# A three-stage kernel (decayed linear attention, routed experts, dense MLP): w, k and r laid out head-dimension first

## The reference

```python
# B, H, S, D = 4, 8, 768, 48
for t in range(S):                              # attention
    cur = einsum('bhd,bhe->bhde', u * k[t], v[t])
    y[t] = einsum('bhd,bhde->bhe', r[t], state + cur)
    state = w[t][..., None] * state + einsum('bhd,bhe->bhde', k[t], v[t])
x = y as (B*S, H*D) = (3072, 384)
# 8 experts: noisy top-2 routing, out += weight * relu(x @ w1[e]) @ w2[e]
# then h = x @ w_in ; out = (h - tanh(h)) @ w_out
```

## Time and profile before

| | us |
|---|---|
| median of 3 runs | 1186.56 (1183.66 to 1186.65) |
| profiled execution, time | 1191.79 |
| profiled execution, span | 1190.3 |
| PE busy | 1104.0 (93%) |
| DVE busy | 738.1 (62%) |
| ACT busy | 567.3 (48%) |
| POOL busy | 136.8 (11%) |

### The profile page before, as it was taken

The page is one execution under the profiler, slowest core; times in us unless marked ns, Lnnn a source line. Parts: engine busy times, 40 slices in busy tenths (PEclk is TensorE's granted clock), DMA queues, the critical chain, the costliest instruction groups (busy, mean ns, idle before and its releaser), DMA issues.

```text
span 1190.3 us, 24896 instructions
## 1 busy us (share of the span) xinstructions
PE 1104.0 (93%) x8968; PEld 1053.2 (88%) x8968; DVE 738.1 (62%) x1036; ACT 567.3 (48%) x808; POOL 136.8 (11%) x188
## 2 busy tenths in 40 slices
PE   5888867789799999999999999999999999999998
PEld 4677756689799999999999999899999999999998
DVE  8999988638957777766677777643434333343433
ACT  5445433346347666666666666532332323333232
POOL 1000223212820000000000000221010101101010
PEclk9999889889999999999999999999999999999999
DMA  9664555556778888888888888511010101101010
GB/s 154 122 123 88 121 117 157 175 189 190 258 245 288 280 278 269 281 277 276 276 273 289 264 276 282 184 47 36 25 60 0 59 0 59 59 0 59 0 59 20
DMA packets 192751, 185.04 MB, mean 155 GB/s; under 512 B 98192, under 2 KB 160912, under 8 KB 192688
## 3 DMA queue, kind: packets, MB, share of 16 engines
q1 hardware_dynamic: 176208, 152.74, 44.8%
q0 software_dynamic: 6528, 20.06, 5.1%
q10 hardware_dynamic: 9952, 11.41, 2.8%
HBM read 156.85 MB, written 27.33 MB: 155 GB/s over the span
## 4 chain that ended last, share of the span: by engine, by line
PE 77%; DVE 13%; issue 5%; ACT 3%; SPq 1%; POOL 1%; DMA 1%; another core or an unknown queue 0%; DVEq 0%; ACTq 0%; POOLq 0%
PE ps L789 6%; PE ps L858 6%; PE ps L876 6%; PE ps L878 6%; PE ps L877 6%; PE ps L859 6%; PE ps L860 6%; PE ps L790 5%; PE ps L791 5%; PE ps L747 5%; PE ps L749 4%; PE ps L748 4%; PE ps L767 2%; PE ps L766 2%; PE ps L765 2%
## 5 line engine op out<-in xcount | busy, mean ns | idle before, releaser
L1590 DVE TENSOR_TENSOR w_lo<-w_raw,w_hi 128x1536 fp32r<-128x1536 f32 x140 | 244.3, 1755 | 93.3 <-ACT w_hi L909 88.1
L909 ACT ACTIVATE w_hi<-w_raw 128x1536 fp32r<-128x1536 f32 x140 | 206.5, 1488 | 24.8 <-ACT y_out L1101 12.3
L1590 DVE TENSOR_TENSOR gg<-ps,th 128x768 f32<-128x768 f32 x64 | 61.3, 957 | 168.3 <-ACT th L1148 168.3
L789 PE MATMUL ps<-w_hi,h_hi 128*128 128x384 f32 x440 | 151.0, 343 | 9.0 <-DVE h_lo L1674 8.3
L747 PE MATMUL ps<-xT_hi,w_hi 128*128 128x256 f32 x480 | 139.6, 291 | 10.9 <-issue 5.7
L791 PE MATMUL ps<-w_hi,h_lo 128*128 128x384 f32 x440 | 147.9, 336 | 0.0
L790 PE MATMUL ps<-w_lo,h_hi 128*128 128x384 f32 x440 | 147.9, 336 | 0.0
L1878 POOL DMA_INDIRECT yy<-yg,slot_g x54 | 54.2, 1004 | 751.3 <-DVE w_lo L1590 425.5
L749 PE MATMUL ps<-xT_hi,w_lo 128*128 128x256 f32 x480 | 137.2, 286 | 0.0
L748 PE MATMUL ps<-xT_lo,w_hi 128*128 128x256 f32 x480 | 137.1, 286 | 0.0
L876 PE MATMUL ps<-wout_hi,g_hi 128*128 128x384 f32 x384 | 130.4, 340 | 0.0
(11 more groups left out here) (266 smaller groups left out, 2088.1 us busy)
## 6 DMA issues: line engine op xcount, KB each, us to landing
w_raw<-in_moe_w SPq DMA_DIRECT2D x140, 768.0 KB
xt_in<-xg SPq DMA_DIRECT2D x20, 384.0 KB
yg<-y_out ACTq DMA_DIRECT2D x20, 384.0 KB
k_pad<-in_k SPq DMA_DIRECT2D x32, 144.0 KB, 3.9
v_nat<-in_v SPq DMA_DIRECT2D x32, 144.0 KB
out<-o_out SPq DMA_DIRECT2D x8, 576.0 KB
w_nat<-in_w SPq DMA_DIRECT2D x15, 288.0 KB, 3.3
r_pad<-in_r SPq DMA_DIRECT2D x30, 144.0 KB
```

The costliest lines, as they stand in the source:

```text
L789: pe.matmul(o, h_hi[:, f, cols], w2_hi[:, f, :], start=(f == 0), stop=False, skip_group_check=True)
L909: nc.scalar.activation(dst, src, ACT.Copy).then_inc(s, 1)
L1590: vec.tensor_tensor(dst, a, b, ALU.subtract).then_inc(s, 1)
```

## The change

The host passes w, k and r a second time with the head dimension before time, and v with the two heads of a pair together. k and r are loaded straight into klin and rlin, w straight into wz, which is now double. `turn`, `straight`, `spread_in`, `squares` and `see` go away. Padding rows of klin and rlin are cleared once by POOL, wz is set to 1 once by DVE.

The scores of a chunk are made in 64-step blocks: the upper-right part that the mask would clear is not computed. DVE masks only the two diagonal 64x64 blocks of each chunk (`mask`, 384 elements a partition into Ad), and ACT copies the off-diagonal one (`apart`, into Ao). `intra` multiplies the diagonal blocks and a new `below` the off-diagonal ones. The betas go to the KV bank. The bonus rows are added on PE, as two matmuls with the identity (`add_bonus`), and ACT instead of DVE copies the finished rows (`tokens`). The range check of w is two Relu instructions on ACT with an accumulated sum (`check_range`). `finish` (the wait for a batch's last rows and the branch to the general path) moves from place 3 of pairs 3, 7 and 11 to place 0 of the next pair. The cast of the first w1 also waits for the last kr.

```diff
+wz = two(place, "wz", [P, Q * W1 + 1])
...
+def load_cols(e, dst, src, landed, n, h):
+    s = n % 2
+    e.dma_start(dst[s][h * HB:h * HB + D, :], src[n // HP, 2 * (n % HP) + h]).then_inc(landed[s], 16)
+
+def load_w(e, n, h):
+    s = n % 2
+    e.dma_start(wz[s][h * HB:h * HB + D, 0:Q * W1].rearrange("d (q s) -> d q s", s=W1)[:, :, 1:W1],
+                w_cols[n // HP, 2 * (n % HP) + h].rearrange("d (q s) -> d q s", s=C)).then_inc(w_in_s[s], 16)
...
 def next_w(n):
 
     if n < NP:
-        sp.wait_ge(spread, n - 1)
-        sp.wait_ge(w_squared, n - 1)
-        load_w(n)
+        sp.wait_ge(scanned, 2 * (n - 2) + 2)
+        sp.wait_ge(w_checked, 2 * (n - 2) + 2)
+        for h in range(2):
+            load_w(sp, n, h)
...
+        c0 = (t * QT + j) * C
+        pe.matmul(ps[0:HB, A0 + h, j * C:(j + 1) * C], kG[s][rows, c0:c0 + HB], rPW[s][rows, c0:c0 + C], start=True, stop=True)
+        mm = pe.matmul(ps[HB:C, A0 + h, j * C:j * C + HB], kG[s][rows, c0 + HB:c0 + C], rPW[s][rows, c0 + HB:c0 + C],
                        start=True, stop=True)
-if t == 0:
-    mm.then_inc(A_full, 1)
+mm.then_inc(A_full, 1)
...
+pe.matmul(ps[rows, KV, BETA + 2 * q:BETA + 2 * q + D], kr[:, q * C + half * HB:q * C + (half + 1) * HB],
+          usel[:, p % HP, :], start=True, stop=True, skip_group_check=True)
...
+                o = (h * QT + q % QT) * HB
+                mm = pe.matmul(ps[rows, Y0 + h, q * D:(q + 1) * D], Ad[q // QT][rows, o:o + HB], v_nat[s][rows, q, h, :],
+                          start=(q == 0), stop=(q == 0), skip_group_check=True)
+    mm.then_inc(diagonal, 1)
+
+def below(p):
+
+    s = p % 2
+    pe.wait_ge(diagonal, p + 1)
+    for q in range(Q):
+        for h in range(2):
+            o = (h * QT + q % QT) * HB
+            mm = pe.matmul(ps[HB:C, Y0 + h, q * D:(q + 1) * D], Ao[q // QT][:, o:o + HB], v_nat[s][0:HB, q, h, :],
+                           start=False, stop=True, skip_group_check=True)
     mm.then_inc(intra_done, 1)
+
+def add_bonus(p):
+
+    pe.wait_ge(bv_done, p + 1)
+    for h in range(2):
+        pe.matmul(ps[:, Y0 + h, 0:Q * D], ident[:], bv[:, :, h, :], start=False, stop=True, skip_group_check=True)
...
 for p in range(NP):
     scores(1, p)
     if p % HP == 2:
         any_bad(p // HP)
     betas(p)
-    back(p)
     step(p, 0)
-    if p + 2 < NP:
-        turn(1, p + 2)
     outer(p)
     step(p, 1)
     intra(p)
     if p + 1 < NP:
         scores(0, p + 1)
+        back(p + 1)
+    below(p)
+    add_bonus(p)
     inter(p)
     step(p, 2)
-    if p + 2 < NP:
-        turn(2, p + 2)
-    if p + 3 < NP:
-        turn(0, p + 3)
     step(p, 3)
...
+def apart(t, p):
+
+    act.wait_ge(A_masked, 2 * p + t + 1)
+    follow(act, intra_done, p)
+    cp(Ao[t][:].rearrange("s (h j t) -> s h j t", h=2, t=HB),
+       ps[0:HB, A0:A0 + 2, 0:QT * C].rearrange("s h (j t) -> s h j t", t=C)[:, :, :, HB:C], A_apart)
+
+def tokens(p):
+
+    b, hp = p // HP, p % HP
+    act.wait_ge(Y_full, p + 1)
+    cp(x_all[b][:, :, hp * PW:(hp + 1) * PW].rearrange("t q (h d) -> t h q d", h=2),
+       ps[0:C, Y0:Y0 + 2, 0:Q * D].rearrange("t h (q d) -> t h q d", d=D), x_done)
...
+act.wait_ge(w_in_s[n % 2], 32 * (n // 2 + 1))
+values = wz[n % 2][:, 0:Q * W1].rearrange("d (q s) -> d q s", s=W1)[:, :, 1:W1]
+for side, sign in ((0, -1.0), (1, 1.0)):
+    follow(act, w_checked, 2 * n + side)
+    nc.scalar.activation(w_out_of[:].rearrange("d (q s) -> d q s", s=C), values, ACT.Relu, bias=limits[:, side:side + 1],
+                         scale=sign, accum_out=over[:, n, side:side + 1]).then_inc(w_checked, 1)
...
 for p in range(NP):
-    keep_back(p)
+    apart(0, p)
+    apart(1, p)
     step(p, 0)
-    straight(1, p + 2)
-    squares(p + 3)
+    chunk_products(p + 2)
     step(p, 1)
-    chunk_products(p + 2)
+    check_range(p + 3)
     step(p, 2)
-    straight(2, p + 2)
-    straight(0, p + 3)
-    spread_in(p + 4)
+    if p + 1 < NP:
+        keep_back(p + 1)
+    tokens(p)
     step(p, 3)
...
+vec.tensor_tensor(Ad[t][:].rearrange("s (h j t) -> s h j t", h=2, t=HB),
+                  ps[0:C, A0:A0 + 2, 0:QT * C].rearrange("s h (j t) -> s h j t", t=C)[:, :, :, 0:HB],
+                  before_h[:].unsqueeze(1).unsqueeze(1).to_broadcast([C, 2, QT, HB]), ALU.mult).then_inc(A_masked, 1)
...
 for p in range(NP):
     if p == 2:
         v_.wait_ge(tidied, TIDIED)
         v_.wait_ge(consts, 16 * (3 + H))
-    mask(0, p)
+    if p > 0:
+        mask(0, p)
     decayed_k(p + 1)
     step(p, 0)
     suffix_scan(p + 2)
     mask(1, p)
+    decayed_r(p + 1)
+    bonus(p)
     if p % HP == 2:
         range_all(v_, p // HP)
-    bonus(p)
     step(p, 1)
-    decayed_r(p + 1)
     states(p)
     step(p, 2)
     prefix_scan(p + 2)
     products(p + 1)
-    see(p + 3)
-    tokens(p)
     step(p, 3)
...
+po.memset(klin[0][:], 0.0).then_inc(zeroed, 1)
+po.memset(rlin[0][:], 0.0).then_inc(zeroed, 1)
...
+v_pairs = inputs["v"].reshape(B, HP, 2, Q, C, D).transpose(0, 1, 4, 3, 2, 5)
+for name, a in [(f"{n}_cols", inputs[n].transpose(0, 1, 3, 2)) for n in "rkw"] + [("v_pairs", v_pairs)]:
+    a = np.ascontiguousarray(a)
```

More of the change, by code:

```diff
@@ L196, in build @@
         badv = place("badv", [P, 8])
+        over = place("over", [P, NP, 2])
         bad_i = place("bad_i", [1, B, 2], I32)
@@ L684, in step @@
                     part()
-            pe.wait_ge(gaps, 1)
-            for which in range(3):
-                turn(which, 0)
-            turn(0, 1)
+            pe.wait_ge(setup, 1)
             scores(0, 0)
-            turn(1, 1)
-            turn(2, 1)
-            turn(0, 2)
+            back(0)
             for p in range(NP):
@@ L905, in _ @@
-            nc.scalar.activation(tick[:, 3:4], minus_mid[:], ACT.Copy)
-            act.wait_ge(gaps, 8)
+                load_cols(act, rlin, r_cols, r_in_s, 0, h)
+            act.wait_ge(wz_set, 6)
+            load_w(act, 1, 1)
+            act.wait_ge(zeroed, 4)
+            for h in range(2):
+                load_cols(act, rlin, r_cols, r_in_s, 1, h)
+            act.wait_ge(restarts, 5)
+            nc.scalar.activation(tick[:, 3:4], limits[:, 0:1], ACT.Relu)
             def cp(dst, src, s):
@@ L909, in cp @@
                 nc.scalar.activation(dst, src, ACT.Copy).then_inc(s, 1)
-            def straight(which, n):
-                if n >= NP:
-                    return
-                t = T_USE["wkr"[which], n]
-                if which == 0:
-                    follow(act, scanned, 2 * n)
-                else:
-                    follow(act, kr_r, n - 1)
-                    follow(act, (kG_r, rPW_r)[which - 1], n - 1)
-                for half in range(2):
-                    act.wait_ge(T_full[half], t + 1)
-                    src = ps[:, TB[half], 0:3 * P]
-                    if which == 0:
-                        dst = wz[:, 0:Q * W1].rearrange("d (q s) -> d q s", s=W1)[:, :, 1 + half:W1:2]
-                        src = src.rearrange("d (q p) -> d q p", q=Q)
-                    else:
-                        dst = (klin, rlin)[which - 1][n % 2][:, half * QT * C:(half + 1) * QT * C]
-                    nc.scalar.activation(dst, src, ACT.Copy).then_inc(T_copied[half], 1)
@@ L1002, in smooth, with first_high @@
                 ins.then_inc(sp_act, 1)
+            def first_high():
+                act.wait_ge(kr_r, NP)
+                for hf in range(2):
+                    w1_high(whole(0), hf)
             def kept(c, *places):
@@ L1538, in decayed_k @@
                     return
-                for half in range(2):
-                    v_.wait_ge(T_copied[half], T_USE["k", n] + 1)
+                v_.wait_ge(k_in_s[n % 2], 32 * (n // 2 + 1))
                 vec.tensor_tensor(c3(kG[n % 2][:]), c3(klin[n % 2][:]), w3(Gz[:])[:, :, 1:W1], ALU.mult).then_inc(kG_r, 1)
@@ L1545, in decayed_r @@
                     return
-                for half in range(2):
-                    v_.wait_ge(T_copied[half], T_USE["r", n] + 1)
+                v_.wait_ge(r_in_s[n % 2], 32 * (n // 2 + 1))
                 v_.wait_ge(scanned, 2 * n + 2)
@@ L1816, in _ @@
                                  pattern=[[1, C]], channel_multiplier=-1))
+            for h in range(2):
+                half = slice(h * HB, (h + 1) * HB)
+                seq(po.affine_select(out=before_h[half, :], in_=ones[half, 0:HB], compare_op=ALU.is_gt, fill=0.0, base=0,
+                                     pattern=[[1, HB]], channel_multiplier=-1))
+            po.memset(klin[1][:], 0.0).then_inc(zeroed, 1)
+            po.memset(rlin[1][:], 0.0).then_inc(zeroed, 1)
             seq(po.iota(part_no[:], pattern=[[0, 1]], base=1, channel_multiplier=1, allow_small_or_imprecise_dtypes=True))
```

252 lines of the change are left out of this document (90 added, 162 removed).

## The result

The changed kernel takes 1200.08 us (median of 4 runs, 1199.52 to 1203.78), the kernel before 1185.83 (median of 4, 1183.66 to 1186.65): ratio 1.0125, 95% interval 1.0106 to 1.0144. It is slower by 1.2%; forecast were 1158.5 us. Its profiled execution took 1203.78 us, its span 1202.3, 12.0 us more than before.

A forecast was written before the change was run, and what follows sets the result against it. DVE, 90% busy, was taken to bound the attention pairs. Savings of 13.8 (pairs 0 to 7), 11 (pairs 8 to 15) and 3.3 (start), 28.1 us off 1191.79, gave 1163.7, as median 1158.5 us; range 1149 to 1178.

The forecast's parts named there:

- The ring: Quiet pairs: PE's list closes on itself through ACT's tokens and apart, 9.0 us in series; scores(1) waits for apart.
- DVE's own loop: Quiet pairs: DVE's work from one first mask to the next falls from 10.46 to 8.63 us.
- TensorE's low and high ends: PE's work per quiet pair, taken at 7.44 us: 6.3 with every low end, 10.4 with every high end.
- `below` ... taken at 0.85 (35 ns each, near intra's 31): PE, each pair: the 24 new off-diagonal instructions cost 0.85 us, within 0.61 to 1.74.
- by columns ... 0.65, which I take: PE, each pair: four bonus instructions of 288 columns cost 0.65 us, scaled from the 128-column row; not below 0.29.
- the 13.8 us: Saving in pairs 0 to 7: 77 us for 90.8, with 9.1 us for a pair without routing.
- rival B: PE and ACT in series become the bound: PE 8.9, ring 10.4 us, total 1177; sign: pace over 10; chance 0.22.
- What is saved comes behind it: Start: after the first scan, work runs without waits for PE or ACT; kG of pair 1 at 17.8, 3.3 us saved.
- In pairs 8 to 15 DVE has two to five us of routing on top and stays the bound: Routed pairs: they save at most 14.6 us, taken at 11 because softplus steps wait behind the later tokens.
- Rival C: Waits and thinned array work keep the clock low in pairs 0 to 7, losing some 17 us: 1200; chance 0.10.
- A: DVE stays the bound everywhere, new PE instructions cost their low ends, ACT's links hide: 35 us saved, 1151; chance 0.13.
- D: Gain given back at the attention stage's end, first expert tile waiting for scattered rows or weights: 1186; chance 0.05.

The follow-up runs named there:

- no_below: Changed kernel without the 24 instructions of `below`, so part of the output is missing: 1182.21 us, ratio 0.9912 to the kernel before.
- no_bonus: Changed kernel without the four bonus instructions on PE, so the output lacks the bonus rows: 1204.84 us, ratio 1.0128 to the kernel before.
- below_mixed: Changed kernel with `below`'s 24 instructions issued four behind every four of the next pair's first scores call: 1225.89 us, ratio 1.0285.
- act_order: Changed kernel with ACT's first Ao copy ahead of tokens and the third range check, softplus ahead of both copies: 1200.65 us, ratio 1.0067.
- whole_scores: Changed kernel with whole 128x128 scores masked whole, no `below` or `apart`; loads, range check and bonus on PE kept: 1172.3 us, ratio 0.9843.
- clock_filler: Changed kernel plus six identity matmuls (12 instructions) a pair where PE waits for Ao: 1209.75 us, ratio 1.0175.
- two runs with filler: clock_filler, and the same six matmuls added to the kernel of opening the ring: 1206.35 us, ratio 1.0113 for the latter.
- opening the ring: act_order with softplus left behind tokens on ACT and DVE's next mask ahead of the router's part: 1199.71 us, ratio 1.0076.
- whole_late: whole_scores with DVE's next mask ahead of the router's part, plus 24 row scatters delayed until the last tokens: 1199.92 us, ratio 1.0064.
- late_scatter: Kernel of opening the ring with the 24 row scatters of the first two batches delayed until the last tokens: 1221.53 us, ratio 1.0235.
- bonus_dve: Changed kernel with the bonus rows added by DVE again in the copy of the tokens: 1218.62 us, ratio 1.0218.
- ring_again: Kernel of opening the ring run once more, unchanged, as control for late_scatter: 1202.27 us, ratio 1.0087.

## Why the prediction was wrong

**Right.** The mask (552 ns for 551), tokens on ACT (656 for 670), `apart` (481 for 490), the Relus (931 for 940), readout 189 each, inside its bounds of 0 and 490 though above the 100 each that were taken. A scores call took 0.92 us for 0.87. The first backward scan began at 6.85 (forecast 7.3) and kG of pair 1 at 17.17 (17.8). The ring was there, with the wait that was named for it, and DVE's own loop of 8.63 us was shown by no_below (8.62 a pair). TensorE's low and high ends come to 6.2 and 10.3 us by the prediction's own terms, not 6.3 and 10.4; nothing rests on it.

**The terms that failed first: `below` and the bonus.** The step "`below` ... taken at 0.85 (35 ns each, near intra's 31)" measured 1.52, 63 ns each, and "by columns ... 0.65, which I take" measured 1.17. `below` lies inside its bounds (0.61 to 1.74); for the bonus only a low one was given. For the bonus a nearer row stood in the earlier trace rows: six transposes of 128x128 on the whole array start 0.78 us ahead of `outer` (35.43 to 36.21), 130 ns each or 1.02 ns a column, and 4 x 288 columns at that price are 1.17 us. The row taken, 72.5 ns for 128 columns, uses half of the array's rows at a time. PE's work is 8.9 us, not 7.44, so the ring is 10.15, not 9.0, and pairs 1 to 7 gain nothing, where most of the 13.8 us was counted. That is rival B up to here, and its sign, a pace over 10 us with PE full, was there. no_below shows the price of `below`: 1.5 us a quiet pair, and 25 to 39 us in all, as the changed kernel's ratio is taken at 1.0125 or 1.024. The bonus's price shows in one pair of no_bonus and is hidden in its total. B's own reason, instructions in one corner of the array, is supported by below_mixed (2.44 us became 1.88), not settled: four corners were never tried with nothing else changed.

**The start.** "What is saved comes behind it", 3.3 us, came true up to the mask, and was lost in pair 0. The load of pair 2's w was seen to be near, and its price was left inside the low end of 1 us saved. But the queue behind it wasn't walked. The one who waited for it was ACT's range check, with `apart` queued behind it and PE behind that: 5.06 us, and by the betas' 1.52 us PE went on at the slower pace. act_order, which turns the two round, has pair 0 at 11.70.

**The routed pairs.** "In pairs 8 to 15 DVE has two to five us of routing on top and stays the bound" is the step that cost most. 11 us were counted as saved; 15.1 were lost in pairs 8 to 14 and 3.4 in the last. DVE did have less to do there, 78.28 us for 90.82 over pairs 8 to 14, and no longer set the pace: PE did, 98.28 us busy where it had been 80.05, and its waits. The range was missed by this more than by anything else. What the runs show of it:

- The blocks make it: whole_scores, without them, takes 98.16 us for these seven pairs, and saves.
- The granted clock is where it is seen. Its mean over pairs 8 to 14 was 0.78 against 0.90, and 0.50 against 0.74 in the last, and at full clock pair 10 took 17.57 us (clock_filler) instead of 21.41. The falls came with idle times of PE, most of them waits for ACT's copy of Ao, which the change had put into PE's path. That the waits bring the clock down is argued from the traces, and two runs with filler support it only in part. Rival C had this mechanism, but in pairs 0 to 7 and as the only cause. That its total, 1200, is the measured one is luck: these pairs and the start lost little, 2.1 us together, pairs 8 to 15 lost 18.4, and 8.6 came back in the expert stage, on which C did not count.
- The ring passes through the router's work: softplus on DVE waits for ACT, which reaches it behind the tokens, and mask and `apart` wait behind softplus. The prediction had seen this and allowed 3.6 us for it (14.6 to 11). It cost PE 4.01 us in pair 10 alone. But opening the ring gave only 4.1 us over pairs 8 to 14 in the traces; most of what it gives lies in pairs 1 to 7.
- PE is starved while GpSimd issues row scatters. Gaps of this kind were there before as well. Where DVE sets the pace the scatters cost 3.8 to 4.7 us over pairs 10 to 14 (whole_late), with PE in the opened ring 20.7 (late_scatter), 16 of it as busy time of PE (71.26 to 55.11) and most of that by the clock. In the changed kernel as it stands their part isn't shown.

How the loss divides among waits, scatters and clock isn't settled: each run that took one away changed the others. bonus_dve and no_bonus fell to the lower clock already in pairs 1 to 4, behind waits of 1.2 to 2.2 us for Ao, while waits of 1.23 us in the changed kernel did not bring it: why the one falls and the other doesn't is open.

**Rivals A and D.** A fell with the ring. D fell too, and with the other sign: the expert stage gave 8.6 us back.

## What to carry to other kernels

When work is taken from the engine that sets the pace and given to one that is 80% busy, price the new instructions by the nearest row of the same place in the array and the same width, not by a mean of kinder rows: here 24 instructions cost 63 instead of 35 ns each and four cost 290 instead of 163, and nearly the whole gain of a quiet pair was gone. Walk every new copy's queue, at the start and in each stage that has extra work, and ask what stands ahead of it. And an engine that becomes the bound takes over every disturbance that its idle time had hidden: here the lower clock, and in the opened ring the row scatters, which cost 4.7 us over five pairs while DVE was the bound and 20.7 with TensorE in the ring.

## What the hardware showed that was not expected

- In ring_again TensorE issued only 3 to 6 instructions every 0.7 to 0.8 us while GpSimd issued row scatters (0.97 to 1.30 us each), with gaps of 0.2 to 0.5 us that have no releaser; `outer` took 3.5 us instead of 0.75. Moved away, the gaps ahead of `outer` and `intra` fell from 8.9 to 1.2 us. By which path the scatters reach TensorE, no run shows.
- 24 fp32 instructions of 64x64 with 48 columns, all on the same 64 rows and 64 columns of the array, took 63 ns each; mixed with others in other quarters, 24 of them and 24 for scores took 39 ns each (1.88 us for 48).
- Four instructions of 128x288 with the identity took 1.17 us, 290 ns each, about 1.0 ns a column; the scores' 72.5 ns for 128 columns gave 0.57 a column, which was no guide: those alternate between two row halves. The full-array transposes of the earlier trace rows, 1.02 ns a column, were.
- Less work for TensorE went with a longer pair: 14.31 us with the bonus on DVE against 10.16 with it on PE, at a mean clock of 0.64 instead of 1.00. After a wait of 2.2 us the clock was 0.50 for ten us although PE was busy all the time.
- Reading out an activation's accumulated sum is an instruction of its own, 189 ns.
